# Gated linear attention and two feed-forward blocks on one core: keys turned ahead of y, keys times values behind it, diagonals and the level of 16 moved between engines

## The reference

```python
B, H, S, D = 4, 8, 768, 48
f = sigmoid(f_logit)
for t in range(S):
    state = f[:, :, t, :, None] * state + einsum('bhd,bhe->bhde', k[:, :, t], v[:, :, t])
    y[:, :, t] = einsum('bhd,bhde->bhe', q[:, :, t], state)
x = y as (B*S, H*D) = (3072, 384)
h = x @ w_in                       # 384 x 2048
g = where(h >= 1, h, where(h <= -1, 0, (h + 1)**2 / 4))
x = g @ w_out                      # 2048 x 384
out = (silu(x @ w_gate) * (x @ w_val)) @ w2_out    # 384 x 1536, 1536 x 384
```

## Time and profile before

| | us |
|---|---|
| median of 3 runs | 1041.23 (1040.88 to 1042.34) |
| profiled execution | 1040.82, span 1039.0 |
| TensorE busy | 988.9 (95%) |
| VectorE busy | 519.5 (50%) |
| ScalarE busy | 450.4 (43%) |
| GpSimd busy | 434.6 (42%) |
| mean granted clock of TensorE | 0.988 |

### The profile page before, as it was taken

How to read it: one execution, slowest core, us unless ns; L and a number is a source line. 1 busy time by engine, 2 the same in 40 slices (tenths; PEclk the granted TensorE clock), 3 DMA queues, 4 the chain that set the end, 5 groups by cost and what they waited for, 6 DMA issues and landing times.

```text
span 1039.0 us, 19480 instructions
## 1 busy us (share of the span) xinstructions
PE 988.9 (95%) x8072; PEld 822.6 (79%) x8072; DVE 519.5 (50%) x644; ACT 450.4 (43%) x800; POOL 434.6 (42%) x362
## 2 busy tenths in 40 slices
PE   4559979999999999999999999999999999999997
PEld 4558768888888888888888888888888888888886
DVE  7999966854964685486346422223222232232221
ACT  5645557657656655865355422222222222221211
POOL 7867734762664475275256211221122112211121
PEclk9979989999999999999999999999999999999999
DMA  9252015006002400400531010010100100000000
GB/s 362 111 186 100 2 42 183 31 3 224 32 2 91 164 3 16 149 32 2 183 122 48 14 61 1 1 61 1 32 29 1 61 1 1 31 1 1 31 1 30
DMA packets 17367, 63.52 MB, mean 61 GB/s; under 512 B 1920, under 2 KB 2176, under 8 KB 16512
## 3 DMA queue, kind: packets, MB, share of 16 engines
q1 hardware_dynamic: 17280, 62.28, 16.5%
HBM read 52.84 MB, written 9.44 MB: 60 GB/s over the span
## 4 chain that ended last, share of the span: by engine, by line
PE 87%; DVE 8%; issue 2%; DMA 1%; ACT 0%; SPq 0%; POOLq 0%; DVEq 0%; ACTq 0%
PE acc L522 11%; PE acc L524 10%; PE acc L523 10%; PE bank L548 7%; PE bank L550 7%; PE bank L549 7%; PE hid L508 6%; PE hid L509 6%; PE hid L510 6%; PE bank L379 4%; DVE scores L856 3%; PE hid L548 2%; PE hid L550 2%; PE hid L549 2%; DVE scores L820 2%
## 5 line engine op out<-in xcount | busy, mean ns | idle before, releaser
L1040 POOL TENSOR_TENSOR g_lo<-prod,g_hi 128x512 fp32r<-128x512 f32 x72 | 93.1, 1293 | 347.3 <-ACT g_hi L745 347.3
L1033 POOL TENSOR_TENSOR g_lo<-act_tmp,g_hi 128x512 fp32r<-128x512 f32 x96 | 127.3, 1327 | 170.9 <-ACT g_hi L706 170.2
L938 DVE TENSOR_TENSOR sig<-sig,bank 128x512 f32<-128x512 f32 x72 | 49.5, 688 | 275.8 <-ACT sig L739 275.8
L745 ACT CAST g_hi<-prod 128x512 fp32r<-128x512 f32 x72 | 44.7, 621 | 248.1 <-PE acc L524 248.1
L1000 POOL TENSOR_TENSOR keys<-keys,gates 128x512 f32<-128x512 f32 x82 | 109.7, 1338 | 71.5 <-PE bank L379 48.5
L508 PE MATMUL hid<-x_hi,win_hi 128*128 128x512 f32 x288 | 116.9, 406 | 9.1 <-DVE act_tmp L926 7.6
L856 DVE COPY_PREDICATED scores<-mask,bank 64x512 f32<-64x512 int32 x120 | 116.4, 970 | 7.9 <-PE bank L379 5.9
L522 PE MATMUL acc<-g_hi,wout_hi 128*128 128x512 f32 x288 | 114.1, 396 | 0.0
L509 PE MATMUL hid<-x_lo,win_hi 128*128 128x512 f32 x288 | 113.1, 393 | 0.0
L510 PE MATMUL hid<-x_hi,win_lo 128*128 128x512 f32 x288 | 113.1, 393 | 0.0
L524 PE MATMUL acc<-g_hi,wout_lo 128*128 128x512 f32 x288 | 112.3, 390 | 0.0
(11 more groups left out here) (86 smaller groups left out, 1853.7 us busy)
## 6 DMA issues: line engine op xcount, KB each, us to landing
gates<-in_f_dram SPq DMA_DIRECT2D x12, 512.0 KB, 5.1
queries<-in_q_dram SPq DMA_DIRECT2D x12, 512.0 KB, 4.7
keys<-in_k_dram SPq DMA_DIRECT2D x12, 512.0 KB, 4.6
values<-in_v_tok_dram SPq DMA_DIRECT2D x6, 1024.0 KB, 7.8
q_tok<-in_q_tok_dram SPq DMA_DIRECT2D x12, 384.0 KB, 8.2
k_tok<-in_k_tok_dram SPq DMA_DIRECT2D x12, 384.0 KB, 8.6
x_dram<-x_out SPq DMA_DIRECT2D x6, 768.0 KB, 3.7
x_raw<-x_dram SPq DMA_DIRECT2D x6, 768.0 KB, 5.6
```

What stands on the lines that cost most here:

```text
L1033: pool.tensor_tensor(g_lo[:, c % RING, :], act_tmp[:, 2 + c % 2, :], g_hi[:, c % RING, :].bitcast(F32), ALU.subtract).then_inc(g_lo_done, 1)
```

## The change

- Order of the bank fills: turned keys, then y, then keys times values. `turn_keys` now comes one visit before y, and `key_values` in y's own visit, right behind it. In the first unit both are issued before the first block (they were inside it).
- Level 16 is taken by ScalarE as plain block copies (`take_blocks`: four copies of 16 rows x 256 a group) instead of by VectorE with a mask.
- The first unit's diagonal is placed by VectorE in four pieces by batch (`place_first`, four predicated copies of 32 x 256 each), and y of a batch waits for its own batch's diagonal alone. Its own products are on VectorE (`own_first`), not GpSimd.
- The second unit's diagonal is placed by ScalarE at places 2 to 5, ahead of the levels.
- The second unit's levels are at places 6, 9, 12, 14, 16 (before 4, 7, 10, 13, 15), its y at 25 (before 23); for the later units y is at 23 (before 21).
- Splits of w_in and w_out move: GpSimd does one of eight w_in splits before the own products of the second unit, three behind, four in chunks 1 to 4; VectorE does one w_out split before the block and seven in it (before four and four).
- Twelve warming products instead of four after the last level. Keys are loaded before queries from the third unit on.
- What waits for what stays as it was, renumbered: a bank fill waits for the taking of the fill three before it (keys times values of group 1 thus for the x_lo of batch 2, in y's order), and ScalarE's first diagonal of a unit waits until all four y of the unit before are written (`act.wait_ge(filled, fill(a - 1, KV0))`).

```diff
--- before.py
+++ after.py
@@ -28,8 +28,9 @@
...
 STEPS = 2 * (NL - 2)
+MASKED = STEPS - 2
 LAG = 2
-WARM, WARM_FROM = 4, 4
+WARM, WARM_FROM, WARM_LAST = 4, 4, 12
@@ -40,14 +41,16 @@
...
 LAST0 = WHOLE0 + 1
-Y0 = LAST0 + 2
-TK0 = Y0 + B
-KV0 = TK0 + B
+TK0 = LAST0 + 2
+Y0 = TK0 + B
+KV0 = Y0 + B
 FILLS = KV0 + 2
-LAST_FILLS = TK0
-DVE_A_UNIT, ACT_A_UNIT = STEPS + 2, 3 + B
+DVE_A_UNIT = MASKED + 2
+ACT_Y = STEPS - MASKED + 3
+ACT_A_UNIT = ACT_Y + B
@@ -57,33 +60,36 @@
...
 H_FIRST = -13
-BY_VECTOR = 2
-Plan = namedtuple("Plan", "own diag place sigmoid gated copy step take scale turn whole whole_take last last_take "
+Plan = namedtuple("Plan", "own diag place sigmoid gated copy step take block_take scale turn whole whole_take last last_take "
                           "decay y y_out tk tk_out kv state state_place")
-FIRST = Plan(own=(19, 19), diag=(21, 22), place=(21, 22), sigmoid=(-6, -5), gated=(-6, -4),
-             copy=(-6, -4, 1, 3, 5, 7, 9, 11, 13, 15, 19, 19), step=(0, 2, 4, 6, 8, 10, 12, 14, 16, 18),
-             take=(2, 4, 6, 8, 10, 12, 14, 16, 18, 20), scale=(-5, 2, 3, 5, 7, 9, 11, 13, 15, 17, 19, 19),
+FIRST = Plan(own=(20, 22), diag=(20, 22), place=(21, 21, 23, 23), sigmoid=(-6, -5), gated=(-6, -4),
+             copy=(-6, -4, 1, 3, 5, 7, 9, 11, 13, 15, 17, 19), step=(0, 2, 4, 6, 8, 10, 12, 14, 16, 18),
+             take=(2, 4, 6, 8, 10, 12, 14, 16), block_take=(18, 20), scale=(-5, 2, 3, 5, 7, 9, 11, 13, 15, 17, 19, 19),
              turn=(0, 2, 4, 6, 8, 10, 12, 14, 16, 18, 20, 20, 22, 22), whole=20, whole_take=21, last=22, last_take=23,
-             decay=24, y=(24, 24, 24, 24), y_out=(24, 24, 25, 25), tk=(HS, HS, HS, HS), tk_out=(HS, HS, HS, HS),
-             kv=HS + 2, state=HS + 3, state_place=HS + 5)
+             decay=24, y=(24, 24, 24, 24), y_out=(24, 24, 25, 25), tk=(23, 23, 23, 23), tk_out=(24, 24, 24, 24),
+             kv=25, state=HS + 1, state_place=HS + 4)
...
     two = [h for h in levels for _ in range(2)]
-    p = Plan(own=(-13, -12), diag=(-12, -11), place=(-9, -8, -6, -4), sigmoid=(-2, -1), gated=(-1, 0),
+    p = Plan(own=(-13, -12), diag=(-10, -9), place=(-8, -7, -5, -3), sigmoid=(-2, -1), gated=(-1, 0),
              copy=[h + g - 2 for h in levels for g in range(2)] + [whole - 1] * 2, step=two,
-             take=[h + g + 1 for h in levels for g in range(2)], scale=two + [whole] * 2 + [last] * 2,
+             take=[h + g + 1 for h in levels[:-1] for g in range(2)], block_take=[levels[-1] + 1, levels[-1] + 2],
+             scale=two + [whole] * 2 + [last] * 2,
              turn=[h + g for h in levels + (whole, last) for g in range(2)], whole=whole, whole_take=whole + 1,
-             last=last, last_take=last + 1, decay=y + 1, y=(y, y, y, y), y_out=(y, y, y + 1, y + 1),
-             tk=(y + 2, y + 2, y + 3, y + 3), tk_out=(y + 3, y + 3, y + 4, y + 4), kv=y + 4, state=y + 5, state_place=HS + 5)
+             last=last, last_take=last + 1, decay=y - 2, tk=(y - 1,) * B, tk_out=(y - 1, y - 1, y, y), y=(y,) * B,
+             y_out=(y, y, y + 1, y + 1), kv=y, state=y + 2, state_place=HS + 5)
...
-SECOND = usual((4, 7, 10, 13, 15), 18, 21, 23, own=(0, 1), diag=(3, 3), place=(19, 20), sigmoid=(-2, -1),
+SECOND = usual((6, 9, 12, 14, 16), 18, 21, 25, own=(-8, -8), diag=(1, 1), place=(2, 3, 4, 5), sigmoid=(-2, -1),
                gated=(-1, 1))
-USUAL = usual((2, 5, 8, 11, 13), 16, 19, 21)
-PLANS = [FIRST, SECOND, USUAL._replace(place=(-8, -7, -5, -4))] + [USUAL] * (UNITS - 3)
+USUAL = usual((2, 5, 8, 11, 13), 16, 19, 23)
+PLANS = [FIRST, SECOND, USUAL._replace(place=(-7, -6, -5, -3))] + [USUAL] * (UNITS - 3)
+W2_SLOTS = (1, 3, 5, 6, 7, 8)
@@ -310,11 +324,12 @@
...
         for a in range(1, UNITS):
-            load_q(a)
             if a == 1:
+                load_q(a)
...
             if a > 1:
+                load_q(a)
...
@@ -322,7 +337,7 @@
...
-        sp.wait_ge(filled, fill(UNITS - 1, LAST_FILLS))
+        sp.wait_ge(filled, fill(UNITS - 1, KV0))
@@ -409,10 +420,10 @@
...
             free(a, i)
+            pe.wait_ge(diag_placed, B * a + b + 1)
             if b == 0:
-                pe.wait_ge(dve_took, a * DVE_A_UNIT + STEPS)
-                pe.wait_ge(act_took, a * ACT_A_UNIT + 3)
-                pe.wait_ge(diag_placed, B * (a + 1))
+                pe.wait_ge(dve_took, a * DVE_A_UNIT + MASKED)
+                pe.wait_ge(act_took, a * ACT_A_UNIT + ACT_Y)
@@ -473,24 +484,23 @@
...
                 if a == 0 and s >= WARM_FROM:
-                    keep_warm()
+                    keep_warm(WARM)
...
                 if a == 0:
-                    keep_warm()
+                    keep_warm(WARM)
...
                 if a == 0:
-                    keep_warm()
+                    keep_warm(WARM_LAST)
+            if a < UNITS - 1:
+                for b in placed(PLANS[a].tk, h):
+                    turn_keys(a, b)
...
                 outputs(a, b)
-            if a < UNITS - 1:
-                for b in range(B):
-                    if PLANS[a].tk[b] == h:
-                        turn_keys(a, b)
-                if h == PLANS[a].kv:
-                    for g in range(2):
-                        key_values(a, g)
+            if a < UNITS - 1 and h == PLANS[a].kv:
+                for g in range(2):
+                    key_values(a, g)
@@ -621,9 +631,21 @@
...
+        def take_blocks(a, g):
+            act.wait_ge(filled, fill(a, MASKED + g + 1))
+            act.wait_ge(dve_took, a * DVE_A_UNIT + MASKED)
+            t = bank[fill(a, MASKED + g) % 3]
+            for n in range(P // Q):
+                r = slice(Q * n, Q * n + Q // 2)
+                o = group(scores, g)[r, :, :, Q * n + Q // 2:Q * (n + 1)]
+                i = t[r, :].rearrange("p (x e b t) -> p x e b t", e=2, b=2, t=Q // 2)[:, :, :, n % 2, :]
+                last = act.copy(o, i)
+            last.then_inc(act_took, 1)
...
             act.wait_ge(filled, fill(a, LAST0))
-            act.wait_ge(dve_took, a * DVE_A_UNIT + STEPS)
+            act.wait_ge(dve_took, a * DVE_A_UNIT + MASKED)
@@ -672,11 +696,12 @@
...
                 copy_right(a, s)
+            if a < UNITS - 1:
+                for b in placed(PLANS[a].tk_out, h):
+                    take_keys(a, b)
...
             if a < UNITS - 1:
-                for b in placed(PLANS[a].tk_out, h):
-                    take_keys(a, b)
@@ -752,8 +777,7 @@
...
             if h in (23, 25):
-                for i in range(2):
-                    split_w2(h - 23 + i)
+                split_w2((h - 23) // 2)
...
@@ -766,8 +790,8 @@
...
                     attention(a, place)
-                if m == 0 and 6 <= c < W2N + 2:
-                    split_w2(c - 2)
+                if m == 0 and c in W2_SLOTS:
+                    split_w2(2 + W2_SLOTS.index(c))
@@ -807,18 +837,19 @@
...
-        def place_diag(a, g):
-            if g == 0:
-                dve.wait_ge(const_in, 16)
-                dve.wait_ge(dve_took, a * DVE_A_UNIT + STEPS)
-            dve.wait_ge(diag_done, 2 * a + g + 1)
+        def place_first(b):
+            dve.wait_ge(const_in, 16)
+            dve.wait_ge(dve_took, MASKED)
+            dve.wait_ge(act_took, STEPS - MASKED)
+            dve.wait_ge(diag_done, b // 2 + 1)
...
                 r = slice(Q * n, Q * (n + 1))
-                d = diag[r, g * BP:(g + 1) * BP].rearrange("p (x a) -> p x a", a=1).broadcast_to([Q, BP, Q])
-                i = eye[r, r].bitcast(I32).rearrange("p (a t) -> p a t", a=1).broadcast_to([Q, BP, Q])
-                o = group(scores, g)[r, :, :, r].rearrange("p x e t -> p (x e) t")
+                d = diag[r, b * H:(b + 1) * H].rearrange("p (x a) -> p x a", a=1).broadcast_to([Q, H, Q])
+                i = eye[r, r].bitcast(I32).rearrange("p (a t) -> p a t", a=1).broadcast_to([Q, H, Q])
+                o = scores[r, b * PAIRS:(b + 1) * PAIRS, :, r].rearrange("p x e t -> p (x e) t")
                 last = dve.copy_predicated(o, i, d)
-            last.then_inc(diag_placed, 2)
+            last.then_inc(diag_placed, 1)
@@ -883,10 +912,12 @@
...
             for g in placed(PLANS[a].diag, h):
+                if a == 0:
+                    own_first(g)
                 sum_own(a, g)
-            if a < BY_VECTOR:
-                for g in placed(PLANS[a].place, h):
-                    place_diag(a, g)
+            if a == 0:
+                for b in placed(PLANS[a].place, h):
+                    place_first(b)
@@ -1007,8 +1039,9 @@
...
         def attention(a, h):
-            for g in placed(PLANS[a].own, h):
-                own(a, g)
+            if a > 0:
+                for g in placed(PLANS[a].own, h):
+                    own(a, g)
@@ -1045,10 +1078,10 @@
...
                 attention(a, place)
-            if h == 20:
+            if h == 23:
                 split_w1(0)
-            elif 23 <= h < 22 + W1N:
-                split_w1(h - 22)
+            elif 25 <= h < 28:
+                split_w1(h - 24)
...
@@ -1057,6 +1090,8 @@
...
```

(39 more changed lines are left out.)

34 lines of the change are left out of this document (14 added, 20 removed).

## The result

The changed kernel takes 1051.23 us (1050.54 to 1052.34, four runs), the kernel before in the same comparison 1041.39: ratio 1.0091 [1.0079, 1.0104], slower. The forecast was 1039.9 with a range of 1030 to 1046, so the time lies outside it. The profiled execution has a span of 1049.3 us against 1039.0: 10.3 us to be found.

What follows compares the result with a forecast made beforehand. TensorE was taken as the bound, busy behind 142 us, so only the start could give time. 1040.8 - 4.5 (comparison point) + 3.2 (visit of y) + 0 (steady state) = 1039.5, 1039.9 beside the median; range 1030 to 1046.

Steps and rivals of the forecast that it cites:

- the first unit: Start of the run: second sum done at 50.6, first hidden chunk near 58.5, second unit's loads only 2 us earlier.
- the idle stretch: Behind hidden chunk 1: TensorE idles from 62.6 to 71.0, until VectorE's activation lets hidden chunk 2 start.
- the lead of 9 us: First hidden chunk: forecast 10 us earlier, a lead not kept because the second unit's loads come only 2 us earlier.
- the rival of whole turns: First unit's diagonal: VectorE and GpSimd take turns whole, second sum at 52.9, 2.3 later, time 1042.2; chance 0.18.
- Gain at the comparison point: 4.5 us: Where chunk 11 is done and only project chunk 9 precedes second unit's y: 135.4 instead of 139.9.
- The diagonal in the chain of copies: Second unit, ScalarE: four diagonal batches of 2.45 us among the copies for level 1, ending at 83.5; TensorE waits 3.4.
- The rival that VectorE is not short: Level 1 to level 32: no TensorE waits, 7.5 us less, 1032.4; chance 0.26 together with no wait at y.
- the visit of y: Second unit's keys times values: third unit's first diagonal precedes batch 2's split on ScalarE, 3.2 us of new idle TensorE.
- slower: Rival: costlier first-diagonal pieces, 1044.7 at 55.4; the 3.4 and 3.2 us holes may lower the clock, 1.9 each; chance 0.16.
- I put the steady state at 0: Third unit on: y at 23, diagonal at 24 behind batch 2's split, keys' copy two banks ahead; no change, 0 us.
- the hole of 7.6 us: Ahead of hidden chunk 11, behind the second unit's diagonal on VectorE: worth 7.6 + 1.9 for the low clock = 9.5 us.

Runs made afterwards that it cites:

- experiment 4: Changed kernel with third unit's diagonal one place later, GpSimd's own products two later, and second unit's queries and gates loaded first: 1040.66 us, ratio 0.9988.
- experiment 3: Also called both: changed kernel with third unit's diagonal one place later and later units' GpSimd own products two places later; 1042.57 us, ratio 1.0016 to the kernel before.
- experiment 6: On top of both, five of eight w_out splits moved ahead of the first block, the rest behind chunks 9, 10 and 12: 1043.48 us, ratio 1.0010.
- experiment 10: On top of experiment 8, the first unit's state placed apart at place 44 instead of 36: 1040.35 us, ratio 0.9979.
- experiment 11: On top of experiment 10, the second batch of the second unit's diagonal moved to place 0, behind the sigmoids: 1040.02 us, ratio 0.9972.
- experiment 2: Changed kernel with GpSimd's own products two places later in the later units and their sums one later: 1047.2 us, ratio 1.0044.
- experiment 8: On top of both, second unit's sums and first two diagonal batches earlier, and w_out splits spread to chunk 14: 1038.3 us, ratio 0.9962.
- experiment 1: Changed kernel with the third unit's diagonal on ScalarE one place later, behind batch 2's split: 1046.18 us, ratio 1.0041.
- experiment 9: Kernel before with the second unit's diagonal on VectorE cut from four instructions a group to one: 1034.95 us, ratio 0.9943.
- Experiment 12: Kernel before with only the second unit's diagonal moved to ScalarE ahead of the levels, own products and sums earlier: 1042.16 us, ratio 0.9999.

## Why the prediction was wrong, step by step

**Right: the first unit.** The second sum was to be done at 50.6, the first hidden chunk to start at 58.5, and the loads to come only 2 us earlier. Timelines after, of VectorE, ScalarE and SyncE's queue:

```profile
43.14 5.11 DVE L851 COPY_PREDICATED scores<-eye,diag 32x256 f32<-32x256 int32 x8
...
51.09 4.08 DVE L851 COPY_PREDICATED scores<-eye,diag 32x256 f32<-32x256 int32 x8
...
64.45 1.52 DVE L825 TENSOR_TENSOR queries<-queries,gates 128x1024 f32<-128x1024 f32 x1 [5.55 <-ACT gates L601]
...
70.27 0.68 DVE L957 TENSOR_TENSOR act_tmp<-hid,act_tmp 128x512 f32<-128x512 f32 x1
```

```profile
36.94 1.49 ACT L643 COPY scores<-bank 16x256 f32<-16x256 f32 x4 [0.28 <-DVE scores L885]
...
63.36 1.06 ACT L601 ACTIVATE gates<-gates 128x1024 f32<-128x1024 f32 x1 [5.19 <-DMA gates<-in_f_dram]
...
75.12 1.68 ACT L682 COPY state_apart<-state 64x768 f32<-64x768 f32 x2
...
81.01 2.44 ACT L612 ACTIVATE scores<-eye,diag 128x128 f32<-128x128 f32 x8
83.36 1.30 ACT L631 COPY right_q<-queries 64x512 f32<-64x512 f32 x2
```

```profile
50.98 0.33 SPq L290 DMA_DIRECT2D q_tok<-in_q_tok_dram  x1
...
53.81 1.30 SPq L272 DMA_DIRECT2D gates<-in_f_dram  x2
```

Four small copies of level 16 took 1.49 (1.5 forecast). SyncE's first load is at 50.98, the first hidden chunk at 59.31, and the activation that ends the idle stretch is done at 70.95 (forecast 71.0). In one place the prediction misread the diff: keys are loaded before queries from the third unit on, not the second; nothing in the sum hung on it. The reader sees more than half of the lead of 9 us vanish in one bracket, 5.19 <-DMA; experiment 4 agrees.

That this execution had its second sum near 50.6, and not where the rival of whole turns put it (52.9), was in part luck. Up to there eleven traces (after, and all experiments on the changed kernel) have the same instructions on VectorE and GpSimd. In six of them the first eight pieces of the diagonal took 4.7 to 5.1 us, and the load that waits for the sum was issued at 50.3 to 51.2. In experiments 3, 6, 10 and 11 the pieces took 5.9 to 7.4 and the load was issued at 52.5 to 53.5; in experiment 2 they took 6.1, started 2 us later as well, and the load was issued at 55.06. VectorE's timeline with both:

```profile
44.10 7.41 DVE L851 COPY_PREDICATED scores<-eye,diag 32x256 f32<-32x256 int32 x8
```

So in five of eleven executions the sum came about where the rival had it or later. That the pieces lose their time to GpSimd's scales of keys fits the rows, but no run takes these away. In experiment 6, too, where GpSimd is busy for 8.3 of 9.6 us beside them, five splits take 1.9 each, twice their 0.95.

**The first step that failed: "Gain at the comparison point: 4.5 us".** The diagonal in the chain of copies was right (83.5 forecast, 84.75 measured), but I had left the two copies of the first unit's state, 1.68 us at place 4 of the block, out of ScalarE's order. From there to level 32 I said 41.5 and it took 43.3: the four w_out splits in it took 1.8 each and not 1.48, and the holes cost clock (the rows with 0.50 above). The sum itself had 4.2 for three splits of 1482 ns, which are 4.4. A last wait of 0.8 for `g_lo` came on top. So the comparison point was 0.2 us early and not 4.5. That takes away the gain; it makes no loss. The rival that VectorE is not short fell with it: level 32 came at 128.02, and the stretch to it shrinks when splits are taken out (experiments 6 and 8).

**Half right: the visit of y.** The wait was forecast at 3.2 and measured at 3.04, by the chain described. Its clock, 2.8 us, I had named under "slower" and not put into the sum. So it is 5.8 instead of 3.2, confirmed by experiment 1.

**The second step that failed, and with the visit of y the loss: "I put the steady state at 0".** The prediction looked there at keys times values, at the two banks of lead of the keys' copy and at level 32, and asked for each whether a bank was free. It did not ask what the keys' copy itself waits for: the decayed state. Before, in the third unit, the decay ran at 232.74 for 0.95 us and the first transposes came at 238.02, over 4 us behind its end, and eight more at 240.95. After, the transposes start at 235.29, ahead of the decay's end at 237.13, and are all in one visit; and the decay, no longer clear of GpSimd's own products, has become long. The visit is short, too: 16 transposes take 1.9 us, which does not cover the wait. Each wait of 1.1 lengthens its visit by 1.4, three of them make 4.3 of the 4.4 us, and experiment 2 takes away just these.

Put right, the sum is 1039.0 - 0.2 + 5.8 + 4.4 = 1049.0 for a span of 1049.3. The forecast was 11.3 us too low: 4.3 in the way to level 32, 2.6 in the clock at y, 4.4 in the steady state. The direction came out wrong because a gain of 4.5 was counted that stood at the end of four waits in a row, each moved a little, while the repeated part, whose every us counts three times, got two sentences.

**Open.** The program's head varies by some us from run to run (the first hidden chunk at 58.2 to 62.4 in kernels that hardly differ there). The pieces of the first diagonal are part of it; what else is, and what decides how they fall, no run shows. So the places of experiments 10 and 11 are not told apart from experiment 8, and differences of one or two us between single traces prove nothing. Experiment 12 shows that the moved diagonal costs at the first level about what it gives ahead of y; why 0.7 us of gain in its trace is nothing in the time is within that spread.

## What to carry to other kernels

When a product is moved earlier in a ring of banks, list for every fill the taker's own waits too (here a copy that waits for another engine's decay), and walk that list once for the unit that repeats before the one that starts. Look also at what used to lie between a producer and its reader: here y, whose 6.3 us had covered a slow order on GpSimd. An engine that takes over work must be read in its order at the new place: here diagonal activations of 2.45 us in front of a split that feeds TensorE made a hole of 3.04 and cost 2.8 more by the low clock behind it. Removing a hole gives only what the next wait behind it leaves: the hole of 7.6 us and its clock were 9.5 us, of which a short diagonal gave 7.0 and a moved one nothing. And where single executions spread by as much as the effect, compare traces whose heads agree.

## What was not expected of the hardware

The length of a hole alone does not tell the clock behind it. After, a hole of 3.04 us inside a dense stretch was followed by a granted clock of 0.50, and so was one of 1.81 us ahead of the hidden chunk at 101.96 (0.70 in the two us from 102, 0.50 from 104 to 106); in experiment 9 a hole of 1.80 us was followed by 1.00, and after, the 2.29 us ahead of level 32 were too (1.00 from 128 to 132). Sixteen 128x128 transposes took 1.93 us, 0.12 each, in fp32. VectorE's predicated copies of 32x256 took 0.64 each in a group of eight beside GpSimd (5.11), 0.51 in the next (4.08), and 0.93 in the trace of both (7.41), where 32x512 had taken 1.89.
